# GpSimd multiplies the first attention's probabilities by their reciprocals, and SP's queue loads the first expert weights

## The reference

```python
# 1: windowed attention, 8 heads of 64; heads 0-3 see the last 32 keys, heads 4-7 every 4th of the last 128
scores = np.where(masks, scale * q @ k.T, -1e9)
attn = np.exp(scores - max);  attn = attn / (attn.sum(-1) + 1e-9);  x = attn @ v
# 2: mixture of 4 causal attentions (wq, wk, wv, wo per expert), the best 2 of 4 by x @ w_gate
out += w[e] * (softmax(causal(q_e @ k_e.T)) @ v_e @ wo_e)
# 3: one of 8 feed-forward experts per token, chosen by argmax of the gate or kept from the token before
out[b, s] = p[e] * (np.maximum(x[b, s] @ w1[e], 0) @ w2[e])
```

## Time and profile before

| what | us |
|---|---|
| median of 3 runs (lowest, highest) | 845.7 (844.21, 846.16) |
| the profiled execution's own time | 846.1 |
| its span, from first to last instruction | 844.4 |
| first period, windowed attention of batch 0 alone | up to 66.8 |
| periods with both attentions | 66.8 to about 359, 97.7 each |
| last period, then routing | to 445, then to 479 |
| layer 3 | 479 to 844 |
| PE busy | 772.6 (91%) |
| DVE, ACT, POOL busy | 322.3, 266.5, 82.5 |

### The profile page before, as it was taken

The page is one execution under the profiler, slowest core; times in us unless marked ns, Lnnn a source line. Parts: engine busy times, 40 slices in busy tenths (PEclk is TensorE's granted clock), DMA queues, the critical chain, the costliest instruction groups (busy, mean ns, idle before and its releaser), DMA issues. The chain is left out here.

```text
span 844.4 us, 12479 instructions
## 1 busy us (share of the span) xinstructions
PE 772.6 (91%) x3835; PEld 490.0 (58%) x3836; DVE 322.3 (38%) x976; ACT 266.5 (32%) x864; POOL 82.5 (10%) x141
## 2 busy tenths in 40 slices
PE   8879989899989999899987999999999999999980
PEld 8767866578656876576553544545445454444540
DVE  3663587256861588323525611112111121121110
ACT  2662677247761578402430020111101111011000
POOL 4110010000100000000001111101001011010111
PEclk8998999899997999889986999999999999999996
DMA  6852253113620222000003211551151551010010
GB/s 148 167 148 71 56 142 98 39 32 78 177 60 16 58 69 101 26 7 1 28 24 125 98 45 39 224 218 37 37 212 50 223 225 38 25 50 19 26 49 7
DMA packets 88815, 69.62 MB, mean 82 GB/s; under 512 B 78334, under 2 KB 78366, under 8 KB 86848
## 3 DMA queue, kind: packets, MB, share of 16 engines
q1 hardware_dynamic: 81120, 44.73, 18.5%
q0 software_dynamic: 7648, 24.29, 8.7%
HBM read 118.12 MB, written 11.27 MB: 153 GB/s over the span
## 5 line engine op out<-in xcount | busy, mean ns | idle before, releaser
L988 PE MATMUL bank<-w_sb,pt 128*128 x352 | 158.4, 593 | 1.3 <-DVE pt L1765 1.3
L1008 PE MATMUL bank<-w_all,raw_all 128*128 x352 | 154.8, 592 | 2.3 <-DVE raw_all L1769 2.3
L1353 ACT ACTIVATE raw_all<-bank 128x512 f32<-128x512 f32 x44 | 26.3, 597 | 270.3 <-PE bank L988 270.3
L1008 PEld LDWEIGHTS bank<-w_all,raw_all 128*128 128x128 f32 x352 | 65.4, 191 | 76.2 <-issue 76.2
L988 PEld LDWEIGHTS bank<-w_sb,pt 128*128 128x128 f32 x352 | 64.0, 192 | 65.2 <-issue 65.2
L1778 DVE TENSOR_SCALAR raw_all<-bank,p_slot 128x512 f32 x22 | 16.5, 751 | 156.6 <-PE bank L1008 149.4
L695 PE MATMUL bank<-stage_b,w_all 128*128 128x288 f32 x256 | 66.9, 409 | 0.0
L1196 ACT ACTIVATE pr<-sm,negmax_a 96x80 f32<-96x80 f32 (+1 forms) x168 | 59.7, 358 | 8.8 <-DVE negmax_a L1387 8.6
L570 POOL DMA_INDIRECT out_dram<-raw_all,idx x25 | 25.4, 1017 | 288.9 <-DVE raw_all L1778 274.5
L695 PEld LDWEIGHTS bank<-stage_b,w_all 128*128 128x128 f32 x256 | 46.7, 190 | 11.2 <-issue 0.4
L1185 ACT COPY w_sb<-bank 128x256 f32<-128x256 f32 (+3 forms) x81 | 34.6, 427 | 44.5 <-PE bank L733 43.9
(11 more groups left out here) (212 smaller groups left out, 1029.6 us busy)
## 6 DMA issues: line engine op xcount, KB each, us to landing
w_sb<-in_moe_w_dram SPq DMA_DIRECT2D x19, 2048.0 KB
w_all<-in_moe_w_dram SPq DMA_DIRECT2D x19, 2048.0 KB
w_sb<-in_moe_w_dram POOLq DMA_DIRECT2D x12, 512.0 KB, 4.2
w_all<-in_moe_w_dram POOLq DMA_DIRECT2D x12, 512.0 KB, 4.1
raw_all<-in_q_dram SPq DMA_DIRECT2D x32, 144.0 KB
raw_all<-in_k_dram SPq DMA_DIRECT2D x32, 144.0 KB
mixture_rows<-y_sb SPq DMA_DIRECT2D x16, 256.0 KB, 2.0
v_dil<-in_v_dram SPq DMA_DIRECT2D x48, 80.0 KB, 2.6
```

What stands on the lines that cost most here:

```text
L988: last = pe.matmul(ps[half], xT[:, c * P:(c + 1) * P], w1_sb[:, bass.ds(buf, 1), c * F + half * HALF:c * F + (half + 1) * HALF].rearrange( ...
L1008: last = pe.matmul(ps[5], hidT[:, n * P:(n + 1) * P], w2_sb[:, bass.ds(buf, 1), n // 4, (n % 4) * D:(n % 4 + 1) * D].rearrange("p o n -> p ...
```

## The change

Two things move.

1. `dve_norm` stops after the reciprocal and raises a new semaphore, `sums_ready`. The multiplication (56 of them, 14 for each batch) is done by POOL in `pool_norm`, which waits for `sums_ready` and raises `normed`. PE's order and its waits on `normed` stay.
2. The first expert weights are issued by SP, without waiting for each piece: four DMAs of 512 KB in each period behind the loads of q and k for the next batch and ahead of the first `store_y`; the third expert's eight after the last store. Each expert has a semaphore of its own. POOL issues none of them.

```diff
+            def first_w1(e):
+                for j in range(NC):
+                    sp.dma_start(w1_sb[:, e, j * F:(j + 1) * F], ...).then_inc(ffw_first[e], 16)
+            def first_w2(e):
...
                 if a + 1 < B:
                     load_qk(sp, a + 1, 1)
+                if m in (0, 2):
+                    first_w1(m // 2)
+                if m in (1, 3):
+                    first_w2(m // 2)
                 if m >= 0:
                     store_y(sp, m, 0)
...
+            sp.wait_ge(y_done, B * NT)
+            sp.wait_ge(lg_done, B)
+            first_w1(NBUF - 1)
+            first_w2(NBUF - 1)
             sp.wait_ge(table_ready, 1)
...
+            def pool_norm(b, G):
...
+                pool.wait_ge(sums_ready, b * GA + G + 1)
+                pool.tensor_tensor(p, p, rec[G % 4][0:M, :].unsqueeze(2).broadcast_to([M, NB, nk]), ALU.mult
+                                   ).then_inc(normed, 1)
             for a in range(B):
+                for G in range(GA - 3):
+                    pool_norm(a, G)
                 for i in range(2):
+                    if i == 1:
+                        pool_norm(a, GA - 3)
                     pool.wait_ge(x_moved_d, a * GA + ENDS[i])
...
                     pool.tensor_copy(XT[:, PAIRS[i][1], :], xa[:, i, :]).then_inc(xa_copied, 1)
-                if a % 2 == 0:
-                    first_w1(a // 2)
-                else:
-                    first_w2(a // 2)
-            pool.wait_ge(y_done, B * NT)
-            first_w1(NBUF - 1)
+                for G in range(GA - 2, GA):
+                    pool_norm(a, G)
             pool.wait_ge(y_stored[0], 16 * 3 * B)
             pool.wait_ge(y_stored[1], 16 * 2 * B)
-            first_w2(NBUF - 1)
...
             link(dve, nc.vector.tensor_scalar(rec[G % 4][0:M, :], sums[G % 4][0:M, :], EPS, None, ALU.add))
-            link(dve, nc.vector.reciprocal(rec[G % 4][0:M, :], rec[G % 4][0:M, :]))
-            p = pr4[G % 4][0:M, 0:NB * nk].rearrange("x (n k) -> x n k", k=nk)
-            nc.vector.tensor_tensor(p, p, rec[G % 4][0:M, :].unsqueeze(2).broadcast_to([M, NB, nk]), ALU.mult
-                                    ).then_inc(normed, 1)
+            nc.vector.reciprocal(rec[G % 4][0:M, :], rec[G % 4][0:M, :]).then_inc(sums_ready, 1)
```

More of the change, by code:

```diff
@@ L226, in build @@
         o_done = sem("o_done")
+        sums_ready = sem("sums_ready")
         normed = sem("normed")
@@ L258, in build @@
         index_ready = sem("index_ready")
-        ffw_first = sem("ffw_first")
+        ffw_first = [sem(f"ffw_first{i}") for i in range(NBUF)]
         ffw_loaded = sem("ffw_loaded")
@@ L364, in _ @@
                                  src[e].rearrange("(c p) n -> p c n", p=P)).then_inc(w_loaded, 16)
+            def first_w1(e):
+                for j in range(NC):
+                    sp.dma_start(w1_sb[:, e, j * F:(j + 1) * F],
+                                 w1[e].rearrange("(p c) f -> p c f", c=NC)[:, j]).then_inc(ffw_first[e], 16)
+            def first_w2(e):
+                for a in range(2):
+                    for h in range(2):
+                        sp.dma_start(w2_sb[:, e, a, 2 * h * D:2 * (h + 1) * D],
+                                     w2[e].rearrange("(a p c) d -> a p (c d)", a=2, c=4)[
+                                         a, :, 2 * h * D:2 * (h + 1) * D]).then_inc(ffw_first[e], 16)
             for a in range(B + 1):
@@ L509, in _ @@
             pool.sem_inc(const_ready, 1)
[L511 to L529, removed]
+            def pool_norm(b, G):
+                i, dil, g, blks = group(G)
+                M, nk = ROWS[dil], KEYS[dil]
+                p = pr4[G % 4][0:M, 0:NB * nk].rearrange("x (n k) -> x n k", k=nk)
+                pool.wait_ge(sums_ready, b * GA + G + 1)
+                pool.tensor_tensor(p, p, rec[G % 4][0:M, :].unsqueeze(2).broadcast_to([M, NB, nk]), ALU.mult
+                                   ).then_inc(normed, 1)
             for a in range(B):
+                for G in range(GA - 3):
+                    pool_norm(a, G)
                 for i in range(2):
+                    if i == 1:
+                        pool_norm(a, GA - 3)
                     pool.wait_ge(x_moved_d, a * GA + ENDS[i])
@@ L982, in hidden @@
                     if isinstance(s, int):
-                        pe.wait_ge(ffw_first, PIECES * 16 * (s + 1))
+                        pe.wait_ge(ffw_first[s], PIECES * 16)
                     else:
```

## The result

The changed kernel takes 853.4 us, median of 8 runs (850.8 to 856.4), against 845.7 for the kernel before on the same chip (8 runs, 843.7 to 846.4): a ratio of 1.010 with the 95% interval 1.008 to 1.012. It is slower by 7.7 us. The profiled execution took 855.3 us (span 853.6), near the upper end of its runs; that of before had 846.1 (span 844.4).

What follows compares the result with a forecast made beforehand. PE, busy 89.88 of 97.20 us in a period, bounds the kernel; in the first period, the chain of groups. 5.8 + 0.8 + 2.2 + 0.6 = 9.4 on 846.1 gives 855.5, as median 855.1; range 850.5 to 861.5.

Steps and rivals of the forecast that it cites:

- The stall at the start: First period, group 0: POOL's product stands behind its constants, so PE's transposes come at 26.05 instead of 20.28: +5.8 us.
- One multiplication on POOL: Each group's product on POOL takes 0.67 or 0.57 us, making probabilities later by 0.26 or 0.21.
- rivals of a dear and of a cheap product: POOL's products cost 1.00 and 0.84: 861.8, chance 0.10; or the cheap end takes 2.5 off: 852.6, chance 0.10.
- The rest of the first period: Behind group 0, nine groups on the chain come later, 2.1 us, less gains at three places: net +0.8 us.
- the three periods: Periods with both attentions: product lateness counts only where PE waited for it, 0.2 us a period, +0.6 in three.
- The clock after the stall: Behind PE's standstill in the first period, another 6.6 us stretch at low clock: +2.2 us; 0 if it stays up.
- The weights: First expert weights issued by SP instead of POOL, 24 DMA issues, none on a path: 0 us.
- the clock that does not fall: Rival: behind the stall dummy products bring PE up again at once; -2.2, 852.9 us, chance 0.25.
- The relief of DVE: Rival: 42 products in three periods free 15 us of DVE and periods shrink; all of it gives 840, chance 0.02.
- The shared port: Rival: POOL's and DVE's reads exclude each other, at group 10 alone; at most 2.0 us in three periods, 857.1, chance 0.05.

Runs made afterwards that it cites:

- the two pairs of experiments: Changed kernel with 18 dummy PE products, 850.5 us, against constants built later, 844.0; kernel before with group 0's added wait and those products, 851.8, against before.
- the weights alone: Changed kernel with all products back on DVE, first expert weights still issued by SP: 842.7 us, 2.8 below the kernel before.
- the constants later: Changed kernel, all 56 products on POOL, but POOL builds the router's constants behind batch 0's products: 844.0 us, 1.5 below before.
- the pair of experiments: Changed kernel with the router's constants built behind batch 0's products, 844.0 us, against changed kernel with all products back on DVE, 842.7 us.
- filled kernel: 18 dummy products on PE ahead of its wait for group 0: changed kernel 850.5 us; kernel before with group 0's product waiting for POOL's constants 851.8 us.
- the second set: One of two sets of 29 runs of the unchanged kernel before; their medians are 845.5 and 845.9 us.
- batch 0 on DVE: Changed kernel with the 14 products of batch 0 on DVE, the other 42 on POOL, weights on SP: 843.9 us, 1.7 below before.
- the stall alone: Kernel before, with DVE's product of group 0 in the first period waiting for POOL's constants: 854.6 us, 9.1 above before.
- the last experiment: Changed kernel with the router's constants built later, and POOL adding a tile of zeros ahead of each product and waiting: 883.0 us, 37 above before.

## Why the prediction came out as it did

The forecast was 855.1, with 850.5 to 861.5 as its range; the median is 853.4. Sign, place and size were right. The terms, by offsets of medians: 6.1 + 3.1 + 1.3 - 2.8 = 7.7, where the prediction had 5.8 + 2.2 + 1.4 + 0 = 9.4. These four are the steps from one kernel to the next, so that they add up to the measured 7.7 by construction; that they do confirms none of them. Each is a difference of two medians whose runs spread over several microseconds.

**The stall at the start: right.** 5.8 was predicted; the transposes came 5.87 later in the trace, and the two pairs of experiments give 6.1 and 5.9. The first product began at 25.43, not at 25.3. PE's gap reads 6.9, not 5.8, because in this execution PE began the last work ahead of it at 18.83 and not at 20.03: the start of the program differs between executions. Without a stall, group 0's transposes come at 20.28 in the profile of before and at 18.89 in that of the weights alone, whose clock was up from 12.9 on; the 5.8 is a difference to one such start.

**One multiplication on POOL: right.** 0.67 and 0.57 were taken from the copy of as many elements read, and 0.666 and 0.597 measured, so neither end of the bounds came true, and with them fell the rivals of a dear and of a cheap product. The price is that of a copy that reads as many elements (692 ns for 576). The estimate of 0.63 for 288 elements from the Trainium skill ("GPSIMD Engine Reference", section 3.1) was near as well; this trace has 0.666, for a second input that is a broadcast.

**The rest of the first period and the three periods: right as far as it can be read.** 0.2 a period was predicted, and 0.22, 0.22 and 0.16 measured. The 0.8 of the first period can't be told from the clock in the changed kernel. The versions with the constants later and with the weights alone have the same clock there, and take 47.1 and 46.7 us from group 0's transposes to the first projection: 0.4. Together the terms were to be 1.4; the pair of experiments gives 1.3, less than the runs of one kernel spread.

**The clock after the stall: the mechanism right, its size and length not.** The prediction had one stretch of 6.6 us at half clock, 2.2 us. In the medians it is 3.1. In the profiled execution, whose mean granted clock is 0.937, it is far more: 0.59 to 33 us, then 0.72 to 76. The single row at the program's start, 6.6 us at 0.50, was no measure of how long it stays down. That the idle PE lowers the clock the pairs of runs show: the stalled and the filled kernel differ only in the dummy products, both filled ones are faster, and the clock stayed up where they left 2.4 us of the gap and came back by 33 where they left 3.8. How long it stays low differs between executions of the same kernel: the runs of after have mean clocks from 0.937 to 0.952, and those at 0.952 take 851 to 852 us, those at 0.937 to 0.940 855 to 856. Low stretches without the gap come on top (above, batch 0 on DVE); 7 of the 29 runs of before in the second set took 851 to 854 us, with a lower mean clock than the rest.

That this execution got 4.6 us back later, at a higher clock than before in the last attention and the routing, is in the trace. From the last projection to layer 3 it takes 117.8 us; the profile with batch 0 on DVE, which has no stall, takes 118.0, that of the stall alone 120.8, and before and both filled kernels 122.4 to 122.5. So it also comes without the stall; what decides it stays open.

**The weights: wrong.** The prediction set them at 0 and looked only for a transfer that is late. None was: the first store of y behind them took 9.6 us to land instead of 5.1, and DVE's copy behind it still waited for PE alone:

```profile
158.58 0.69 DVE L1369 COPY y_sb<-bank 128x512 f32<-128x512 f32 x1 [0.32 <-PE bank L770]
```

This answers to the earlier trace rows, 15.4 us later. The step that failed is "POOL loses 24 DMA issues, none on a path": 24 issues fewer on POOL make the program's end shorter by 1.9 us. That was in the trace of before as 9.0 us from the last issue to the end of the span, of which the transfer itself needs about two, and I read nothing there. The remaining 0.9 us of the 2.8 is not accounted for; in the profiled execution the other differences are stretches at another clock (the third period 96.5 us at 0.98, where before has 98.8 at 0.95).

**The rivals.** The time of the clock that does not fall, 852.9, happens to be nearer to the median than the forecast, but the trace refutes the case itself. The range ends at 861.5, just short of the dear product's own 861.8. The errors have opposite signs: 0.9 too little for the clock, 0.3 too little for the stall, 2.8 too much for the weights and 0.1 for the products. Together they took the forecast 1.7 us too high; that they cancel in part is luck. The relief of DVE: 22 us less work, and PE's periods did not shrink.

The shared port: it shows just where the prediction placed it, at group 10, where DVE's two scalings of the second attention run beside POOL's product. Before, then after:

```profile
129.70 0.86 DVE L1464 TENSOR_SCALAR heads_out<-heads_out,inv,gate 128x384 f32<-128x384 f32 x2
```

```profile
144.71 1.19 DVE L1468 TENSOR_SCALAR heads_out<-heads_out,inv,gate 128x384 f32<-128x384 f32 x2
144.86 0.73 POOL L537 TENSOR_TENSOR pr<-pr,rec 96x240 f32<-96x240 f32 x1 [2.48 <-DVE rec L1403]
```

0.33 us more on DVE, in each of the three periods, and 0.73 on POOL where such a product takes 0.58 undisturbed. PE does not wait for it, as forecast: its products that need the scalings start 2.43 us behind the projection of y (L763, L770) ahead of them in both kernels.

## What to carry to other kernels

Before a step goes to an idle engine, look at what stands in that engine's queue ahead of its first use: here constants that were first read some 430 us later held up the first product, at several times the price of 56 slower products (9.2 us against 1.3), and building them later removed the loss. A stall of the engine that sets the end is to be priced with the clock behind it, here half as much again by the medians, and filling the gap with dummy work is a test of that share. A walk by slack, as made here, gives the time in which the engine stands; when the delays grow, the clock that falls with them has to be added.

## What the runs showed of the chip that I had not expected

- A gap of 6.9 us on PE is followed by some 50 us at a mean granted clock of 0.68, although PE was busy 51 of these 56 us. Without the gap the same work ran at 0.95 to 0.97. A stretch of low clock also came without such a gap: 0.66 from 110 to 130 us in the profile with batch 0 on DVE, where PE was busy 19.2 of these 20 us.
- The end of the program, from the last issue on POOL on, took 7.0 to 7.1, 7.8 and 9.0 us with 0, 8 and 24 pieces of 512 KB issued by POOL hundreds of microseconds earlier.
- On POOL a product of two inputs, the second one a broadcast of three values a row, costs 666 ns for 128x288 and 597 for 96x240; an addition of two full tiles in the last experiment costs 792 and 703.
- DVE's scalings and POOL's product, when they overlap, lengthen each other: 1.19 instead of 0.86 us for the pair on DVE, 0.73 instead of 0.58 on POOL.
- Four pieces of 512 KB issued together from SP's queue took 6.3 us from issue to landing in the median of all twelve of w1, against 4.2 one after the other.
